# An attention kernel with two MLP layers: the flag of an all-masked row moves from GpSimd to VectorE

## The chip, the cores and the metric

The program runs on one core of a Trainium2 chip. The core has four engines that compute: TensorE multiplies and transposes matrices, VectorE and ScalarE read the results and work on rows, and GpSimd works on the core's memory beside them. SyncE issues transfers. The metric is the device time of one execution in microseconds (us).

## The reference

What is computed, in order: attention over 4 × 8 heads, 576 positions and 64 columns, in which each row keeps only the scores within `tau` of its maximum, and then two MLP layers over 2304 tokens.

```python
def _attn_ref(q, k, v, tau):
    scale = 1.0 / np.sqrt(q.shape[-1])
    scores = scale * np.matmul(q, k.transpose(0, 1, 3, 2))
    thresh = np.max(scores, axis=-1, keepdims=True) - tau
    scores = np.where(scores >= thresh, scores, -1000000000.0)
    scores = scores - np.max(scores, axis=-1, keepdims=True)
    attn = np.exp(scores)
    attn = attn / (np.sum(attn, axis=-1, keepdims=True) + 1e-09)
    return np.matmul(attn, v).astype(np.float32)

def _moe_ref(x, w_in, w_out, s, b):     # 512 -> 2048 -> 512
    h = x @ w_in
    r = np.maximum(h, 0.0)
    return (s * (r * r) + b) @ w_out

def _moe2_ref(x, w_in, w_out, alpha):   # 512 -> 2048 -> 512
    h = x @ w_in
    g = np.maximum(h, 0.0) + alpha * np.minimum(h, 0.0)
    return g @ w_out
```

A row in which nothing passes the threshold would be a row of equal weights in the reference, since all its scores are then the same. The kernel covers that case with a flag: where the sum of a row is zero, a small number is added to each of its entries before the division.

## The kernel before

The program has three stages: attention, then the first and the second MLP layer. Each engine has a program of its own in one block, and semaphores tie them together. There is no scheduler: the order on each engine is the order in which its code is written.

**Attention** goes over 16 pairs of heads. A pair has 9 tiles of 128 query rows by 576 keys: tile 0 to 7 belong to one head each, even ones to the first and odd ones to the second, and tile 8 holds the last 64 rows of both. `LAYOUT = ["Q", 0, 1, "K", 2, 3, "L", 4, 5, 6, 7, 8]` gives the 12 positions of a pair: at "Q" and "K" the next pair's q and k are transposed, at "L" the last tile of the pair before. `steps` calls each engine's `emit` once per position; pairs 0, 1, 14 and 15 are written out, pairs 2 to 13 run in a loop of two pairs. In the loop the counts that waits compare with are computed in registers of the engine.

A tile passes through five steps. TensorE puts its scores into one of three double banks (`fill`). VectorE takes the negated row maximum (`row_max`, line 788). ScalarE computes the exponentials into `ex` (`exp`, line 616), GpSimd the threshold (`threshold`, line 537). VectorE masks the exponentials with the threshold and sums each row into `rsum` (`mask`, line 796); its semaphore `freed` gives the double bank back to TensorE. For every two tiles (and for tile 8 alone), VectorE adds the guard to the sums (`denominator`, line 802, `den`), inverts them (`invert`, line 807, `rinv`), and GpSimd computes the flag (`all_masked`, line 544, `none_in`). GpSimd then normalises each tile in place (`normalise`, line 550), three positions behind the scores. TensorE transposes the normalised tiles (line 1038, tails in 1035, the last tile in 1046), ScalarE copies them out (line 638), and TensorE multiplies them with v (lines 1072 and 1067). VectorE and ScalarE also split q and k into a high and a low part (`qk_low`, line 814, and line 627).

`all_masked` waits for two things: that the normalisation nine tiles earlier is done, because it overwrites a column of `none_in` that this one read, and that the masking which closes the pair of tiles is done. `normalise` waits for the flag (`none_ok`) and for the inverse (`rinv_ok`). `wait` attaches a wait to the instruction that follows; `wait_alone` puts it on an instruction of its own, which also counts up the semaphore `tick`.

At one position GpSimd normalises, then computes the next threshold, then the flag. VectorE takes the next row maximum, the denominator, a low part of q or k where there is one, masks, and inverts.

The MLP layers follow from some 293 us on. They don't use `none_in`.

Of the kernel before, what the change touches and what calls it, by code (L numbers as in the profile page):

```python
# [28 lines left out]
ALU = mybir.AluOpType  # L29
# [3 lines left out]
P = 128  # L33
# [4 lines left out]
def attention_mlp_mlp(nc, q, k, v, tau, w_in1, w_out1, s, b, w_in2, w_out2, alpha, out):  # L38
    B, H, S, D = q.shape
# [10 lines left out]
    FULL = 2 * (QT - 1)  # L50
    TPP = FULL + 1
# [15 lines left out]
    with ExitStack() as whole, ExitStack() as attention_memory:  # L67
        def sb(name, shape, dt=F32, where=whole):
            return where.enter_context(nc.sbuf_tensor(name, shape, dt))

        def sem(name):
            return whole.enter_context(nc.semaphore(name))
# [39 lines left out]
        none_in = sb("none_in", [P, TPP], where=att)  # L112
        rsum = sb("rsum", [P, TPP], where=att)
# [42 lines left out]
        freed = sem("freed")  # L156
# [5 lines left out]
        none_ok = sem("none_ok")  # L162
        den_ok = sem("den_ok")
        rinv_ok = sem("rinv_ok")
        normed = sem("normed")
# [23 lines left out]
        def wait(eng, sm, value):  # L189

            if not (isinstance(value, int) and value <= 0):
                eng.wait_ge(sm, value)

        def wait_alone(eng, sm, value):

            if not (isinstance(value, int) and value <= 0):
                eng.wait_ge(sm, value)
                eng.sem_inc(tick, 1)
# [10 lines left out]
        GUARD = 1e-9  # L209
# [41 lines left out]
        WEIGHTS += [("in2", j) for j in range(FC)]  # L251
        WEIGHTS += [("out2", j) for j in range(FC)]
        STAGED = [m for m, (kind, _) in enumerate(WEIGHTS) if kind != "in1"]

        def split(kind, j):
# [93 lines left out]
        def last_tile(i):  # L349

            return Use(FINAL - 1, POS + LAYOUT.index(i))
# [10 lines left out]
        def steps(eng, emit):  # L362


            for l in range(-5, BODY):
                emit(0, l)
            with eng.Fori(1, PAIRS // 2 - 1) as it:
                for l in range(BODY):
                    emit(it * 2, l)
            for l in range(BODY):  # L370
                emit(PAIRS - 2, l)
# [136 lines left out]
        @block.gpsimd  # L508
        def _(pool):
            nc.gpsimd.memset(ident[:], 0.0).then_inc(ident_ok, 1)  # L510
            pool.wait_ge(ident_ok, 1)
            nc.gpsimd.affine_select(out=ident[:], in_=ident[:], compare_op=ALU.not_equal, fill=1.0, base=0,
                                    pattern=[[-1, P]], channel_multiplier=1).then_inc(ident_ok, 1)
            nc.gpsimd.memset(q_diag_lo[:].bitcast(F32), 0.0).then_inc(diag_padded, 1)
            pool.wait_ge(tau_in, DMA)
            nc.gpsimd.tensor_scalar(ntau_c[:], tau_c[:], -1.0, 0.0, ALU.mult, ALU.add).then_inc(consts_ok, 1)
            pool.wait_ge(consts_ok, 1)

            def split_lo(m):
                kind, j = WEIGHTS[m]  # L520
                pool.wait_ge(w_hi_ok, m + 1)
                if kind[:2] == "in":
                    chunk = win_lo[:, :, j * P:(j + 1) * P]
                    src = win_raw[:, :, j * P:(j + 1) * P]
                    if kind == "in2":
                        src = stage[:, STAGED.index(m) % 4, :].rearrange("p (c f) -> p c f", c=DC)
                    nc.gpsimd.tensor_tensor(chunk, src, win_hi[:, :, j * P:(j + 1) * P].bitcast(F32),
                                            ALU.subtract).then_inc(w_ok, 1)
                else:
                    nc.gpsimd.tensor_tensor(wout_lo[:, j, :], stage[:, STAGED.index(m) % 4, :],  # L530
                                            wout_hi[:, j, :].bitcast(F32), ALU.subtract).then_inc(w_ok, 1)

            def threshold(t):

                r, c = slice(0, P), t.col
                wait_alone(pool, maxed, t.count + 1)
                nc.gpsimd.tensor_scalar(thr[r, c], negm[r, c], -1.0, ntau_c[r, :], ALU.mult, ALU.add).then_inc(thr_ok, 1)

            def all_masked(t):

                r, c = slice(0, P), t.cols
                wait_alone(pool, normed, t.count - TPP + 1)
                wait_alone(pool, freed, t.uses + 1)
                nc.gpsimd.tensor_scalar(none_in[r, c], rsum[r, c], 0.0, GUARD / S, ALU.is_le, ALU.mult).then_inc(none_ok, 1)

            def normalise(t):
                r, c = slice(0, P), t.col
                wait_alone(pool, none_ok, t.twos + 1)
                wait_alone(pool, rinv_ok, t.twos + 1)
                nc.gpsimd.tensor_scalar(t.ex, t.ex, none_in[r, c], rinv[r, c], ALU.add,  # L550
                                        ALU.mult).then_inc(normed, 1)

            def emit(n0, l):
                before, after, normed_now = Use(n0, l - 1), Use(n0, l + 1), Use(n0, l - NORM_LAG)
                if normed_now.tile:
                    normalise(normed_now)
                if after.tile:
                    threshold(after)
                if before.tile and before.closes:
                    all_masked(before)  # L560

            steps(pool, emit)
            all_masked(last_tile(FULL))
            normalise(last_tile(FULL - 2))
            for m in range(IN1_AHEAD):
                split_lo(m)
            pool.wait_ge(o_out, 2 * PAIRS)
            for m in range(IN1_AHEAD, len(WEIGHTS)):
                split_lo(m)
# [214 lines left out]
        def _(dve):  # L784
# [14 lines left out]
            def denominator(t):  # L799
                r, c = slice(0, P), t.cols  # L800
                wait(dve, freed, t.uses + 1)
                nc.vector.tensor_scalar(den[r, c], rsum[r, c], GUARD, None, ALU.add).then_inc(den_ok, 1)

            def invert(t):
                r, c = slice(0, P), t.cols
                wait(dve, den_ok, t.twos + 1)
                nc.vector.reciprocal(rinv[r, c], den[r, c]).then_inc(rinv_ok, 1)  # L807
# [19 lines left out]
            def emit(n0, l):  # L827
                before, t, after = Use(n0, l - 1), Use(n0, l), Use(n0, l + 1)
                if after.tile:
                    row_max(after)  # L830
                if before.tile and before.closes:
                    denominator(before)
                if t.prepares:
                    qk_low(t)
                if t.tile:
                    mask(t)
                if before.tile and before.closes:
                    invert(before)

            steps(dve, emit)  # L840
            denominator(last_tile(FULL))
            invert(last_tile(FULL))
            for t in (last_tile(FULL - 1), last_tile(FULL)):
                dve.wait_ge(none_ok, t.twos + 1)
# [360 lines left out]
```

## Time and profile before

| | us |
|---|---|
| median of 3 runs | 1107.29 |
| lowest and highest | 1106.79, 1107.41 |
| the profiled execution | 1107.03 |
| its span, first to last instruction | 1105.1 |
| TensorE busy in the span | 1090.8 (99%) |
| VectorE busy | 525.6 (48%) |
| ScalarE busy | 507.9 (46%) |
| GpSimd busy | 258.0 (23%) |

The granted TensorE clock is 0.998 of full over the span. A busy share is a mean over stages that differ: in attention four engines are in use at once, in the MLP layers TensorE is nearly alone. Starts are counted from the first instruction of the span. The row of an instruction ends with the idle time of its engine before it and what ended that, where there was one. Matrix products overlap, so gaps of TensorE show in the rows of its weight loads (PEld) rather than in those of its products (PE). VectorE's rows overlap by some 0.08 us too: a row's duration reaches beyond the start of the next one.

### The profile page before, as it was taken

How to read it: one execution, taken by the hardware profiler on the slowest of the kernel's cores; microseconds unless marked ns; L12 is line 12 of the kernel's file. 1: busy time of each engine (PE TensorE's matmuls, PEld its weight loads, DVE VectorE, ACT ScalarE, POOL GpSimd, SP SyncE). 2: the span in 40 equal slices, each digit the busy share in tenths (PEclk: the TensorE clock that was granted, in tenths of full speed). 3: DMA queues.
4: the chain of work that ended last, by engine and by line, in shares of the span. 5: the costliest groups of instructions: out<-in, count | busy, mean ns of one | idle time of the engine just before them, and what ended most of it. 6: DMA issues, size and time to landing. Idle time of an engine off the chain costs nothing.

```text
span 1105.1 us, 18966 instructions
## 1 busy us (share of the span) xinstructions
PE 1090.8 (99%) x5826; PEld 892.2 (81%) x5826; DVE 525.6 (48%) x1016; ACT 507.9 (46%) x946; POOL 258.0 (23%) x438
## 2 busy tenths in 40 slices
PE   8999999999999999999999999999999999999998
PEld 7777877777688888888888889888888888888897
DVE  7888889888643332242242246522322332332232
ACT  4777878777654332232232235544433333333343
POOL 3566656566564300000000004322000000000000
PEclk9999999999999999999999999999999999999999
DMA  8666566664121100000000003311100100010010
GB/s 188 153 157 154 141 150 149 153 146 123 31 58 48 48 1 1 1 0 0 0 0 0 0 10 96 86 48 29 39 0 0 38 0 0 0 38 0 0 39 20
DMA packets 86554, 59.28 MB, mean 54 GB/s; under 512 B 49376, under 2 KB 69872, under 8 KB 86512
## 3 DMA queue, kind: packets, MB, share of 16 engines
q1 hardware_dynamic: 83248, 57.58, 20.5%
q10 hardware_dynamic: 3264, 1.18, 0.5%
q8 instruction: 22, 0.36, 0.1%
q14 instruction: 20, 0.16, 0.1%
HBM read 30.94 MB, written 4.72 MB: 32 GB/s over the span
## 4 chain that ended last, share of the span: by engine, by line
PE 93%; DVE 2%; ACT 2%; issue 1%; DMA 0%; POOL 0%; SPq 0%; ACTq 0%; POOLq 0%; DVEq 0%
PE psum L938 23%; PE psum L940 23%; PE psum L939 23%; PE psum L1072 6%; PE psum L1038 5%; PE psum L967 3%; PE psum L969 3%; PE psum L951 2%; PE psum L1067 2%; DVE act_r L874 2%; PE psum L1046 1%; ACT win_hi L593 1%; PE psum L1035 1%; ACT act_r L706 0%; DMA k_twice<-k_hi 0%
## 5 line engine op out<-in xcount | busy, mean ns | idle before, releaser
L940 PE MATMUL psum<-x_hi,win_lo 128*128 128x512 f32 (+1 forms) x640 | 238.7, 373 | 0.0
L939 PE MATMUL psum<-x_lo,win_hi 128*128 128x512 f32 (+1 forms) x640 | 238.2, 372 | 0.0
L938 PE MATMUL psum<-x_hi,win_hi 128*128 128x512 f32 (+1 forms) x640 | 238.1, 372 | 0.0
L939 PEld LDWEIGHTS psum<-x_lo,win_hi 128*128 128x128 f32 x640 | 120.2, 188 | 24.0
L938 PEld LDWEIGHTS psum<-x_hi,win_hi 128*128 128x128 f32 x640 | 120.3, 188 | 23.0
L940 PEld LDWEIGHTS psum<-x_hi,win_lo 128*128 128x128 f32 x640 | 120.2, 188 | 22.9
L885 DVE SCALAR_TENSOR_TENSOR act_r<-act_n,nalpha,act_r 128x512 f32<-128x512 f32 (+1 forms) x80 | 56.2, 702 | 160.1 <-ACT act_r L717 159.8
L874 DVE SCALAR_TENSOR_TENSOR act_r<-act_r,s_c 128x512 f32<-128x512 f32 (+1 forms) x80 | 72.4, 905 | 116.4 <-ACT act_r L706 116.4
L616 ACT ACTIVATE ex<-psum,negm 128x576 f32<-128x576 f32 x144 | 107.5, 747 | 37.9 <-DVE negm L788 36.7
L709 ACT ACTIVATE g_hi<-act_r,b_c 128x512 fp32r<-128x512 f32 (+1 forms) x80 | 54.6, 682 | 152.5 <-PE psum L940 122.4
L550 POOL TENSOR_SCALAR ex<-ex,none_in,rinv 128x576 f32<-128x576 f32 x142 | 117.5, 828 | 19.9 <-DVE rinv L807 13.0
L796 DVE SCALAR_TENSOR_TENSOR ex<-psum,thr,ex 128x576 f32<-128x576 f32 x144 | 117.1, 813 | 8.8 <-ACT ex L616 3.7
L788 DVE TENSOR_REDUCE negm<-psum 128x1 f32<-128x576 f32 x144 | 107.8, 748 | 25.7 <-PE psum L969 24.1
L877 DVE SCALAR_TENSOR_TENSOR g_lo<-act_r,b_c,g_hi 128x512 fp32r<-128x512 f32 (+1 forms) x80 | 56.4, 704 | 133.6 <-ACT g_hi L709 133.6
L938 PE MATMUL psum<-g_hi,wout_hi 128*128 128x512 f32 (+1 forms) x320 | 118.1, 369 | 1.0 <-DVE g_lo L877 1.0
L940 PE MATMUL psum<-g_hi,wout_lo 128*128 128x512 f32 (+1 forms) x320 | 118.1, 369 | 0.0
L939 PE MATMUL psum<-g_lo,wout_hi 128*128 128x512 f32 (+1 forms) x320 | 117.7, 368 | 0.0
L940 PE MATMUL psum<-wout_hi,g_lo 128*128 128x512 f32 x288 | 112.6, 391 | 0.0
L938 PE MATMUL psum<-wout_hi,g_hi 128*128 128x512 f32 x288 | 112.4, 390 | 0.0
L939 PE MATMUL psum<-wout_lo,g_hi 128*128 128x512 f32 x288 | 112.2, 390 | 0.0
L888 DVE TENSOR_TENSOR g_lo<-act_r,g_hi 128x512 fp32r<-128x512 f32 (+1 forms) x80 | 51.1, 639 | 105.8 <-ACT g_hi L720 105.8
L716 ACT ACTIVATE act_n<-psum 128x512 f32<-128x512 f32 (+1 forms) x80 | 44.3, 554 | 120.7 <-PE psum L940 120.7
(93 smaller groups left out, 1614.7 us busy)
## 6 DMA issues: line engine op xcount, KB each, us to landing
k_twice<-k_hi SPq DMA_DIRECT2D x64, 144.0 KB, 2.5
stage<-in_moe_w_out_dram SPq DMA_DIRECT2D x32, 256.0 KB, 2.6
out_dram<-stage SPq DMA_DIRECT2D x18, 256.0 KB, 2.2
q_both<-q_hi SPq DMA_DIRECT2D x32, 128.0 KB, 2.3
q_both<-q_lo SPq DMA_DIRECT2D x32, 128.0 KB, 2.3
win_raw<-in_moe_w_in_dram SPq DMA_DIRECT2D x16, 256.0 KB, 2.9
stage<-in_moe_w_in_dram SPq DMA_DIRECT2D x16, 256.0 KB, 2.6
raw_q<-in_q_dram SPq DMA_DIRECT2D x30, 128.0 KB, 2.4
```

What stands on the lines that cost most here:

```text
L550: nc.gpsimd.tensor_scalar(t.ex, t.ex, none_in[r, c], rinv[r, c], ALU.add, ALU.mult).then_inc(normed, 1)
L616: nc.scalar.activation(t.ex.rearrange("p (a c) -> p a c", a=2), t.wide[r, :, 0:HALF], ACT.Exp, bias=negm[r, t.col]).then_inc(exped, 1)
L788: nc.vector.tensor_reduce(negm[r, t.col], t.wide[r, :, 0:HALF], AX.XY, ALU.max, negate=True).then_inc(maxed, 1)
L796: nc.vector.scalar_tensor_tensor(out=e, in0=t.wide[r, :, 0:HALF], scalar=thr[r, t.col], in1=e, op0=ALU.is_ge, op1=ALU.mult, accum_out=rsum ...
L874: nc.vector.scalar_tensor_tensor(out=r, in0=r, scalar=s_c[:], in1=r, op0=ALU.mult, op1=ALU.mult).then_inc(t_ok, 1)
L877: nc.vector.scalar_tensor_tensor(out=g_lo[:, j % 2, 0:n], in0=r, scalar=b_c[:], in1=g_hi[:, j % 2, 0:n].bitcast(F32), op0=ALU.add, op1=ALU ...
L885: nc.vector.scalar_tensor_tensor(out=r, in0=act_n[:, j % 2, 0:n], scalar=nalpha[:, j:j + 1], in1=r, op0=ALU.mult, op1=ALU.add).then_inc(t_ ...
L938: nc.tensor.matmul(dst, lhs[0], rhs[0], start=first, stop=False)
L939: nc.tensor.matmul(dst, lhs[0], rhs[1], start=False, stop=False)
L940: return nc.tensor.matmul(dst, lhs[1], rhs[0], start=False, stop=final)
L1038: mm = nc.tensor.transpose(t.buf[:, c, :], ex[:, t.keys0 + c * P:t.keys0 + (c + 1) * P], ident[:])
L1072: nc.tensor.matmul(o_bank[part, o_cols], raw_v[:, par, h, c, :], pt[:, h, c, cols], start=(c == 0), stop=False)
```

## The change

The flag is computed by VectorE, right behind the denominator, instead of by GpSimd at the end of its position. The operation, its inputs and its shape stay: 128 × 2 elements, or 128 × 1 for tile 8. Both waits move with it.

```diff
@@ -536,13 +536,6 @@
-            def all_masked(t):
-
-                r, c = slice(0, P), t.cols
-                wait_alone(pool, normed, t.count - TPP + 1)
-                wait_alone(pool, freed, t.uses + 1)
-                nc.gpsimd.tensor_scalar(none_in[r, c], rsum[r, c], 0.0, GUARD / S, ALU.is_le, ALU.mult).then_inc(none_ok, 1)
-
...
                     threshold(after)
-                if before.tile and before.closes:
-                    all_masked(before)
 
             steps(pool, emit)
-            all_masked(last_tile(FULL))
             normalise(last_tile(FULL - 2))
@@ -801,6 +791,13 @@
+            def all_masked(t):
+
+                r, c = slice(0, P), t.cols
+                wait_alone(dve, normed, t.count - TPP + 1)
+                wait(dve, freed, t.uses + 1)
+                nc.vector.tensor_scalar(none_in[r, c], rsum[r, c], 0.0, GUARD / S, ALU.is_le, ALU.mult).then_inc(none_ok, 1)
+
...
                 if before.tile and before.closes:
                     denominator(before)
+                    all_masked(before)
                 if t.prepares:
                     qk_low(t)
...
             denominator(last_tile(FULL))
+            all_masked(last_tile(FULL))
             invert(last_tile(FULL))
```

VectorE, at the end of a pair inside the loop, before the change: the masking of tile 7, the denominator of tiles 6 and 7, the masking of tile 8, the inverse, then the next pair's row maximum of tile 0, the denominator of tile 8 and the low part of q. REGISTER_ALU and ISA are instructions of the engine's queue alone.

```order
L796 SCALAR_TENSOR_TENSOR ex,rsum<-psum,thr,ex 128x576 [waits thr_ok,exped]
L802 TENSOR_SCALAR den<-rsum 128x2 [waits freed]
L197 REGISTER_ALU
L796 SCALAR_TENSOR_TENSOR ex,rsum<-psum,thr,ex 128x576 [waits thr_ok,exped]
L192 REGISTER_ALU
L807 RECIPROCAL rinv<-den 128x2 [waits den_ok]
L192 ISA
L788 TENSOR_REDUCE negm<-psum 128x1 [waits filled]
L802 TENSOR_SCALAR den<-rsum 128x1 [waits freed]
L192 ISA
L814 SCALAR_TENSOR_TENSOR q_lo<-psum,q_hi 128x576 [waits qk_hi_ok]
```

The same place with the change (its line numbers are those of the changed file):

```order
L786 SCALAR_TENSOR_TENSOR ex,rsum<-psum,thr,ex 128x576 [waits thr_ok,exped]
L792 TENSOR_SCALAR den<-rsum 128x2 [waits freed]
L197 REGISTER_ALU
L799 TENSOR_SCALAR none_in<-rsum 128x2 [waits normed,freed]
L197 REGISTER_ALU
L786 SCALAR_TENSOR_TENSOR ex,rsum<-psum,thr,ex 128x576 [waits thr_ok,exped]
L192 REGISTER_ALU
L804 RECIPROCAL rinv<-den 128x2 [waits den_ok]
L192 ISA
L778 TENSOR_REDUCE negm<-psum 128x1 [waits filled]
L792 TENSOR_SCALAR den<-rsum 128x1 [waits freed]
L799 TENSOR_SCALAR none_in<-rsum 128x1 [waits normed,freed]
```

Between the denominator and the masking of tile 8 there are now the flag with its two waits and one more register instruction, and the flag of tile 8 stands before the low part of q.

GpSimd at the same place before the change: the normalisation of tile 5, the flag of tiles 6 and 7, the normalisation of tile 6, the next pair's threshold of tile 0, the flag of tile 8, the normalisation of tile 7.

```order
L550 TENSOR_SCALAR ex<-ex,none_in,rinv 128x576 [waits none_ok,rinv_ok]
L197 REGISTER_ALU
L197 REGISTER_ALU [waits normed]
L544 TENSOR_SCALAR none_in<-rsum 128x2 [waits freed]
L197 REGISTER_ALU
L550 TENSOR_SCALAR ex<-ex,none_in,rinv 128x576 [waits none_ok,rinv_ok]
L197 ISA
L537 TENSOR_SCALAR thr<-negm,ntau_c 128x1 [waits maxed]
L197 REGISTER_ALU [waits normed]
L544 TENSOR_SCALAR none_in<-rsum 128x1 [waits freed]
L550 TENSOR_SCALAR ex<-ex,none_in,rinv 128x576 [waits none_ok,rinv_ok]
```

With the change:

```order
L543 TENSOR_SCALAR ex<-ex,none_in,rinv 128x576 [waits none_ok,rinv_ok]
L197 REGISTER_ALU
L543 TENSOR_SCALAR ex<-ex,none_in,rinv 128x576 [waits none_ok,rinv_ok]
L197 ISA
L537 TENSOR_SCALAR thr<-negm,ntau_c 128x1 [waits maxed]
L543 TENSOR_SCALAR ex<-ex,none_in,rinv 128x576 [waits none_ok,rinv_ok]
```

The three normalisations have only the threshold between them now.

## Rows read from the trace of the kernel before

**Rows 1.** Windows: length, busy of PE, PEld, DVE, ACT, POOL, clock, DMA share, GB/s.

```profile
140.00:180.00 40.00, 39.69 (x288) 30.85 (x286) 35.19 (x88) 30.41 (x58) 24.26 (x52) 1.00 0.62 149
...
400.00:1105.00 705.00, 700.08 (x3317) 582.74 (x3315) 233.21 (x336) 239.47 (x448) 41.54 (x32) 1.00 0.06 17
```

**Rows 2.** Timeline, ScalarE copy of the last turned tile: start, duration, engine, line.

```profile
36.23 0.59 ACT L643 COPY pt<-psum 128x512 f32<-128x512 f32 x1 [1.09 <-PE psum L1046]
...
265.30 0.59 ACT L643 COPY pt<-psum 128x512 f32<-128x512 f32 x1 [1.05 <-PE psum L1046]
```

**Rows 3.** Waits of weight loads, 60 to 260 us: total, times, longest.

```profile
PEld psum L1038 <- issue: 4.1, 12, 0.4
```

**Rows 4.** Timeline of one period's end, 147.3 to 155.7 us, all engines.

```profile
147.39 0.76 DVE L788 TENSOR_REDUCE negm<-psum 128x1 f32<-128x576 f32 x1 [0.92 <-PE psum L969]
...
148.13 0.81 DVE L796 SCALAR_TENSOR_TENSOR ex<-psum,thr,ex 128x576 f32<-128x576 f32 x1
...
148.94 0.74 DVE L788 TENSOR_REDUCE negm<-psum 128x1 f32<-128x576 f32 x1
149.00 0.53 PEld L951 LDWEIGHTS psum<-ident,raw_q 128*128 128x128 f32 x5 [0.22 <-DVE ex L796]
...
149.24 0.82 POOL L550 TENSOR_SCALAR ex<-ex,none_in,rinv 128x576 f32<-128x576 f32 x1 [0.32 <-DVE rinv L807]
...
149.59 0.81 DVE L796 SCALAR_TENSOR_TENSOR ex<-psum,thr,ex 128x576 f32<-128x576 f32 x1
...
149.71 0.74 ACT L616 ACTIVATE ex<-psum,negm 128x576 f32<-128x576 f32 x1
150.15 0.26 POOL L537 TENSOR_SCALAR thr<-negm,ntau_c 128x1 f32<-128x1 f32 x1
...
150.40 0.83 POOL L550 TENSOR_SCALAR ex<-ex,none_in,rinv 128x576 f32<-128x576 f32 x1
150.45 0.17 DVE L802 TENSOR_SCALAR den<-rsum 128x2 f32<-128x2 f32 x1
...
150.66 0.82 DVE L796 SCALAR_TENSOR_TENSOR ex<-psum,thr,ex 128x576 f32<-128x576 f32 x1
...
151.48 0.74 DVE L788 TENSOR_REDUCE negm<-psum 128x1 f32<-128x576 f32 x1
...
152.19 0.75 DVE L814 SCALAR_TENSOR_TENSOR q_lo<-psum,q_hi 128x576 fp32r<-128x576 f32 x1
...
152.77 0.27 POOL L537 TENSOR_SCALAR thr<-negm,ntau_c 128x1 f32<-128x1 f32 x1
...
152.92 0.74 DVE L788 TENSOR_REDUCE negm<-psum 128x1 f32<-128x576 f32 x1
...
153.12 0.23 POOL L544 TENSOR_SCALAR none_in<-rsum 128x1 f32<-128x1 f32 x1
...
153.33 0.82 POOL L550 TENSOR_SCALAR ex<-ex,none_in,rinv 128x576 f32<-128x576 f32 x1
...
153.75 0.77 ACT L616 ACTIVATE ex<-psum,negm 128x576 f32<-128x576 f32 x1
154.25 0.27 POOL L537 TENSOR_SCALAR thr<-negm,ntau_c 128x1 f32<-128x1 f32 x1
...
154.42 0.42 PEld L1038 LDWEIGHTS psum<-ident,ex 128*128 128x128 f32 x4 [0.35 <-issue]
...
154.66 0.82 DVE L796 SCALAR_TENSOR_TENSOR ex<-psum,thr,ex 128x576 f32<-128x576 f32 x1 [0.26 <-POOL thr L537]
...
155.56 0.19 PEld L967 LDWEIGHTS psum<-k_twice,q_both 128*128 128x128 f32 x1
```

**Rows 5.** The flag's tile `none_in`: count, duration in ns least, median and greatest.

```profile
L544 POOL TENSOR_SCALAR none_in<-rsum x80: 218/219/238, 16.1 to 292.5; 128x2 f32<-128x2 f32 x64, 128x1 f32<-128x1 f32 x16
```

**Rows 6.** Timeline, tiles 6 and 7 of pair 1, written out without the loop.

```profile
44.67 0.17 DVE L802 TENSOR_SCALAR den<-rsum 128x2 f32<-128x2 f32 x1
...
44.80 0.82 DVE L796 SCALAR_TENSOR_TENSOR ex<-psum,thr,ex 128x576 f32<-128x576 f32 x1
```

## The prediction

> **What bounds the kernel now.** I read the windows by stage first, then the starts that give the attention period, the waits of the weight loads, and one period instruction by instruction. The windows split the span in two [rows 1]. After 400 us, in the two MLP layers, TensorE is busy for 700 of 705 us and nothing that the edit touches runs any more. The edit acts only in attention, up to some 293 us. There VectorE is busy 35.2 of 40 us, ScalarE 30.4, GpSimd 24.3, and TensorE is shown as busy for 39.7, although its weight loads, which show the gaps better, fill 30.9.
>
> Attention repeats once per pair of heads: the copies of the last turned tile start at 36.23 and 265.30 us, with twelve between them, so 13 periods last 229.07 us, 17.62 us each [rows 2]. The waits of the weight loads name a wait of 4.1 us in 12 times, 0.34 each, before transposes of line 1038, put down to "issue" [rows 3]. I take it for a wait on GpSimd: the normalisation of tile 7 runs from 153.33 to 154.15, and the load starts 0.27 us later, at 154.42 [rows 4]. Before the q transposes at 149.00 TensorE waits 0.22 us for a masking on VectorE.
>
> So four engines lean on each other, and a cost on any counts only as far as it reaches TensorE. VectorE is the one with least room: between the row maximum of tile 7 at 147.39, which waited 0.92 us for TensorE, and the masking of tile 1 of the next pair at 154.66 no row of it carries an idle time [rows 4].
>
> **What is taken away.** 80 GpSimd instructions of 219 ns [rows 5], 17.5 us of an engine with room. On the path it matters in one place: the flag of tile 8 at 153.12 stands between the threshold at 152.77 and the normalisation of tile 7 at 153.33. Without it the latter follows the threshold by 0.25 us, as at 150.15 and 150.40, so at 153.02: 0.31 us earlier. The normalisations of tiles 4 and 6 wait for rinv (the row at 149.24 says so) and gain nothing from it; those of tile 2 may, but no wait of TensorE hangs on them. What would TensorE do with 0.31 us? It would start tile 7's transposes earlier, then the scores of tiles 2 and 3. But the bank for tile 3 comes free only when tile 1 is masked, 154.66 + 0.82 = 155.48; with the 0.06 us from such an end to the load (tile 6's masking ends at 148.94, the q load starts at 149.00) that allows 155.54, and the load of tile 3 starts at 155.56. **The gain is 0.02 us per pair**, because the masking of tile 1 waits for the exponential as much as for GpSimd: that ends at 153.75 + 0.77 = 154.52, and the threshold at 154.25 + 0.27 = 154.52 too.
>
> **What is added.** 80 VectorE instructions of the shape of den, and before each a separate wait on `normed` with its count. That wait asks for the normalisation nine tiles back, while GpSimd runs three uses behind: it will find it done. What counts is the time that the next VectorE instruction loses. In a period there are five places.
> - Flags of tiles 4 and 5. The row max takes 0.74 us from its start to the next start where den lies between (147.39 to 148.13), 0.65 where it doesn't (148.94 to 149.59); 0.02 of it is the longer row max. A small instruction queued behind a long one costs **0.07 us**.
> - Flag of tile 8, before q_lo: 151.48 to 152.19 is 0.71, so **0.06 us**.
> - Flags of tiles 6 and 7. Here den is not queued: it waits for the masking of tile 7 (149.59 to 150.40), starts at 150.45, and the masking of tile 8 starts only at 150.66, **0.21 us** later. The data were there sooner: the exponential of tile 8 ends at 150.45, the threshold at 150.41, and at tile 1 the masking followed both 0.14 us after their end. In the part written out without a loop the same pair of starts is 0.13 apart [rows 6]; in the loop the order has a register instruction between. I read the 0.21 as the time in which VectorE's queue works through register, wait and masking once den has let it go, with no long instruction to cover it. The flag brings one more register instruction, one more wait and itself, the same form. Bounds: 0 if only data held the masking back, 0.21 if the row repeats. I take **0.21**, the row nearest in form; 0.13 where no register is computed.
> - Tiles 2 and 3: between den and rinv, which has to wait for den anyway; nothing. Tiles 0 and 1: 0.07, swallowed by VectorE's next wait for TensorE.
>
> **The path, in the loop.** The row max of tile 7 stays at 147.39, it starts with TensorE. Everything after it moves by 0.07, from tile 8's masking on by 0.28 (150.94), and from q_lo on by 0.34. So the row max of tile 1 ends at 153.66 + 0.34 = 154.00, and its exponential, which ScalarE started at 153.75 behind its own queue, starts 0.03 us after that (as 149.71 behind 149.68): 154.03, 0.28 later. The masking of tile 1 follows, 154.94, frees the bank at 155.76, and tile 3's load starts at 155.82 in place of 155.56: **+0.26 us per pair**. The k transposes start later by up to 0.34 too, since q_lo (152.19 + 0.75 = 152.94) holds their bank. But behind them lie the 0.35 us of waiting for tile 7, and these take it up: the normalisation of tile 7 moves by 0.28 with rinv and by 0.31 the other way. From tile 3 on TensorE's stream is gapless or waits for work that it started itself, so that the 0.26 stays until the next period.
>
> **Sum.** The loop holds the ends of pairs 2 to 13: 12 × 0.26 = 3.1. The written-out ends of pairs 1 and 14: 0.07 + 0.13 + 0.06 − 0.08 = 0.18 each, 0.4 (the 0.08 is what ScalarE's queue and the bank leave: 0.34 against 0.26). The end of pair 0 is free, VectorE waits for TensorE there. At the end of attention the exponential of the last tile moves by 0.07. With rounding **+3.5 us**: span 1105.1 to 1108.6, its own run 1107.03 to 1110.6; the run shown lies 0.3 under the median 1107.29, hence **1110.8**.
>
> **Rivals.**
> - *The flag hides in the queue* (nothing at tiles 6 and 7). For it: in all other places register and wait instructions are not seen. Against: 0.21 in the loop, 0.13 outside. Then 0.07 + 0.06 = 0.13 reaches the row max of tile 1, 0.07 its exponential, 0.05 TensorE; 14 × 0.05 + 0.07 = 0.8: 1108.1.
> - *The relief of GpSimd pays.* If ScalarE could start tile 1's exponential some 0.2 us sooner, TensorE would win up to the 0.2 us by which tile 7 comes sooner once VectorE's own 0.13 is paid: 14 × 0.2 = 2.8, 1104.5. It decides from the point where that exponential ends before 154.3. Against it: ScalarE's rows from 149.71 to 154.52 touch each other.
> - *Each flag costs its full slot*, 0.21 in all three places, queued or not: 0.63 − 0.08 = 0.55 a pair, 14 × 0.55 = 7.7: 1115.
> - *The flag and the normalisation exclude each other.* If VectorE had to wait for a normalisation under way, tiles 6 and 7 would lose until 151.23, and tile 8 about 0.5: some 1.07 a pair, 15 us, 1122. Against it: den, the same operation and shape, starts at 150.45 inside the normalisation of 150.40 and takes 0.17, the normalisation 0.83 in place of 0.82. No row shows that den runs in the mode that the flag would run in, so a little chance stays. The Trainium skill has this as a rule (SBUF — State Buffer, "Who interferes with whom"): a VectorE tensor_scalar can take both ports, and then it or the GpSimd instruction, whichever comes second, blocks fully. By that rule the time would be this rival's; the row of den speaks against it here.
>
> **Chances.** Forecast 0.51, hidden 0.27, relief pays 0.07, full slot 0.12, exclusion 0.03. What a measurement of this kernel can tell from no change is about 0.2%, 2.2 us: under 1105.1 is faster, over 1109.5 slower. The forecast case has its own range of 1109.3 to 1111.5, with 0.04 under the line. Slower 0.47 + 0.12 + 0.03 = 0.62; same 0.27 + 0.04 = 0.31; faster 0.07. The range takes in the hidden case with its spread and the lower half of the full slot, 1107.3 to 1113.5, and leaves 0.07 below and about 0.1 above.
>
> **What will show it.** Period 17.88 in place of 17.62; den of tiles 6 and 7 to masking of tile 8 0.4 in the loop, den to masking of tile 6 0.14; the wait before tile 7's transposes near zero; a wait of a load of line 967 for a masking at tile 3, some 0.3 us; GpSimd 17.5 us less busy; the part after 300 us unchanged in length. If the 0.4 reads 0.21, the hidden case holds; if ScalarE's exponential of tile 1 moves by less than VectorE's row max, the price is smaller than summed. A longer normalisation beside a flag would speak for exclusion.

## The result, and the profile after

The changed kernel takes 1111.56 us in the median of 5 runs (1111.47 to 1112.21), against 1107.29 before: a ratio of 1.0042, 95% interval 1.0031 to 1.0052, so it is slower by some 4.3 us. Its profiled execution has a span of 1109.8 us, 4.7 more than that of before. Of the runs below one of e5's five took 1788.52 us, at a granted clock of 0.556; without it the median of e5 would be 1111.7 in place of 1111.91.

The part behind attention did not change. The conversion of x that opens it starts at 299.20 us and the span ends 810.6 us later; before the same two were 294.54 and again 810.6 apart. So all of the difference lies in the attention pairs. The windows of after (columns as in [rows 1]) show the move in the first stretch: VectorE 0.9 us busier in 40, GpSimd 2.8 less, while TensorE and ScalarE lose share because the period got longer.

```profile
140.00:180.00 40.00, 39.32 (x286) 30.56 (x286) 36.07 (x98) 29.87 (x57) 21.47 (x40) 1.00 0.63 151
400.00:1105.00 705.00, 704.00 (x3335) 586.30 (x3334) 234.95 (x339) 241.01 (x450) 41.57 (x32) 1.00 0.05 17
```

The period is read from the starts of q_lo on VectorE, one per pair: 17.63 us before (12 periods of 17.60 to 17.71), 17.99 after (all 13 between 17.97 and 18.02). That is **+0.36 us a pair** where the prediction had +0.26. The same twelve periods make 4.3 of the 4.7 us; at their start q_lo already comes 0.4 us later than before, from the first pairs.

The tiles of the small instructions come next: line, engine, operation and count, then least, median and greatest duration in ns. The flag itself is a 160 ns instruction on VectorE, never longer than 165. But `den`, which the change doesn't touch, has a greatest duration of 706 ns, where it was 172 before.

```profile
L799 DVE TENSOR_SCALAR none_in<-rsum x80: 134/160/165, 14.8 to 297.6; 128x2 f32<-128x2 f32 x64, 128x1 f32<-128x1 f32 x16
L792 DVE TENSOR_SCALAR den<-rsum x80: 133/158/706, 14.7 to 297.5; 128x2 f32<-128x2 f32 x64, 128x1 f32<-128x1 f32 x16
```

Here is the timeline of the period's end that answers to [rows 4]; row 149.37 is the row maximum of tile 7, at 147.39 before.

```profile
149.37 0.76 DVE L778 TENSOR_REDUCE negm<-psum 128x1 f32<-128x576 f32 x1 [1.07 <-PE psum L968]
...
150.04 0.16 DVE L792 TENSOR_SCALAR den<-rsum 128x2 f32<-128x2 f32 x1
150.11 0.16 DVE L799 TENSOR_SCALAR none_in<-rsum 128x2 f32<-128x2 f32 x1
150.18 0.81 DVE L786 SCALAR_TENSOR_TENSOR ex<-psum,thr,ex 128x576 f32<-128x576 f32 x1
...
152.09 0.27 POOL L537 TENSOR_SCALAR thr<-negm,ntau_c 128x1 f32<-128x1 f32 x1
...
152.34 0.83 POOL L543 TENSOR_SCALAR ex<-ex,none_in,rinv 128x576 f32<-128x576 f32 x1
...
152.49 0.69 DVE L792 TENSOR_SCALAR den<-rsum 128x2 f32<-128x2 f32 x1
...
153.09 0.16 DVE L799 TENSOR_SCALAR none_in<-rsum 128x2 f32<-128x2 f32 x1
...
153.16 0.81 DVE L786 SCALAR_TENSOR_TENSOR ex<-psum,thr,ex 128x576 f32<-128x576 f32 x1
...
154.26 0.84 POOL L543 TENSOR_SCALAR ex<-ex,none_in,rinv 128x576 f32<-128x576 f32 x1 [1.10 <-DVE rinv L804]
...
154.63 0.14 DVE L792 TENSOR_SCALAR den<-rsum 128x1 f32<-128x1 f32 x1
154.69 0.14 DVE L799 TENSOR_SCALAR none_in<-rsum 128x1 f32<-128x1 f32 x1
154.75 0.74 DVE L811 SCALAR_TENSOR_TENSOR q_lo<-psum,q_hi 128x576 fp32r<-128x576 f32 x1
...
155.48 0.73 DVE L778 TENSOR_REDUCE negm<-psum 128x1 f32<-128x576 f32 x1
155.54 0.64 PEld L950 LDWEIGHTS psum<-ident,raw_k 128*128 128x128 f32 x6 [0.51 <-DVE q_lo L811]
...
156.25 0.74 ACT L606 ACTIVATE ex<-psum,negm 128x576 f32<-128x576 f32 x1 [0.29 <-DVE negm L778]
...
157.02 0.82 DVE L786 SCALAR_TENSOR_TENSOR ex<-psum,thr,ex 128x576 f32<-128x576 f32 x1
...
157.90 0.19 PEld L966 LDWEIGHTS psum<-k_twice,q_both 128*128 128x128 f32 x1
```

Three readings. The den of tiles 6 and 7 (row 152.49) starts 0.15 us after the normalisation of tile 5 (152.34) and lasts 0.69 us: it ends at 153.18, and the normalisation at 153.17. Before, it started 0.05 us after it, and took 0.17 [rows 4]. One-column den and flag of tile 8 (154.63, 154.69) lie deeper still, 0.37 and 0.43 us, in the normalisation of 154.26 and take 0.14. And the wait of the weight loads before tile 7's transposes, 0.34 us a pair in [rows 3], has gone; the loads now wait for q_lo before the k transposes (row 155.54).

How far each step came from tile 7's row maximum, before and after: masking of tile 8 3.27 and 3.79 (+0.52); q_lo 4.80 and 5.38 (+0.58); row maximum of tile 1 5.53 and 6.11 (+0.58); its exponential 6.36 and 6.88 (+0.52); its masking 7.27 and 7.65 (+0.38); tile 3's load 8.17 and 8.53 (+0.36).

The traces hold one more place where the two engines meet, at the very end of attention, where VectorE normalises two tiles of 128 × 576 itself while GpSimd normalises a third. First the kernel before, then the changed one:

```profile
292.60 1.07 DVE L846 TENSOR_SCALAR ex<-ex,none_in,rinv 128x576 f32<-128x576 f32 x2
292.74 1.46 POOL L550 TENSOR_SCALAR ex<-ex,none_in,rinv 128x576 f32<-128x576 f32 x1
```

```profile
297.77 1.13 POOL L543 TENSOR_SCALAR ex<-ex,none_in,rinv 128x576 f32<-128x576 f32 x1 [1.10 <-DVE rinv L804]
297.79 1.42 DVE L845 TENSOR_SCALAR ex<-ex,none_in,rinv 128x576 f32<-128x576 f32 x2
```

A VectorE row stands for both of its instructions. Before, VectorE starts 0.14 us ahead: its two take 0.58 each, and GpSimd's takes 1.46 in place of 0.82. After, GpSimd's recorded start is 0.02 ahead: VectorE's first takes 0.58 all the same and GpSimd's 1.13; VectorE's second, 0.52 behind GpSimd's start, takes 0.93. So the two engines already held each other up in the kernel before, once, and either can be the one that is held.

### The profile page after: what moved, and what is told of

The parts are those of the page before. It is cut to its first block, busy times and chain, and to the rows that moved or that the text cites. A ratio compares the mean times of both kernels' runs of the same rounds, so it can differ in the third digit from the quotient of the medians.

```text
span 1109.8 us, 18826 instructions
## 1 busy us (share of the span) xinstructions
PE 1093.1 (99%) x5826; PEld 893.5 (81%) x5826; DVE 535.9 (48%) x1096; ACT 508.7 (46%) x946; POOL 240.1 (22%) x358
## 4 chain that ended last, share of the span: by engine, by line
PE 85%; DVE 6%; issue 4%; ACT 1%; SPq 1%; DVEq 1%; DMA 0%; POOL 0%; ACTq 0%; POOLq 0%
PE psum L939 23%; PE psum L937 23%; PE psum L938 23%; PE psum L1071 6%; PE psum L966 3%; PE psum L968 2%; PE psum L1066 2%; DVE act_r L873 2%; PE psum L1037 2%; DVE ex L786 1%; PE psum L950 1%; DVE negm L778 1%; PE psum L1045 1%; DVE q_lo L811 1%; ACT win_hi L583 1%
```

## The experiments

Two theories stood after this. **Hold** (exclusion in the expectations)**:** a two-column tensor_scalar of VectorE that starts well inside a normalisation on GpSimd is held until that ends; the 0.52 us is this. **Queue:** the flag's register and wait instructions on VectorE cost what the prediction said, and den's length only covers them. The table has all kernels; the period is the mean from the q_lo starts, the ratio is to the kernel before on the same chip.

| kernel | median us (runs) | ratio (95%) | period us |
|---|---|---|---|
| after | 1111.56 (5) | 1.0042 (1.0031 to 1.0052) | 17.99 |
| e1_den_single | 1111.40 (5) | 1.0040 (1.0026 to 1.0055) | 17.96 |
| e2_both_single | 1111.95 (4) | 1.0043 (1.0026 to 1.0060) | 17.98 |
| e3_no_flags | 1108.55 (10) | 1.0015 (1.0005 to 1.0024) | 17.79 |
| e4_spare_on_vector | 1114.27 (4) | 1.0066 (1.0049 to 1.0083) | 18.13 |
| e5_no_normed_wait | 1111.91 (5) | 1.0044 (1.0028 to 1.0060) | 17.98 |
| e6_behind_mask | 1112.25 (4) | 1.0047 (1.0030 to 1.0064) | 18.01 |
| e7_single_no_wait | 1107.65 (10) | 1.0006 (0.9996 to 1.0016) | 17.69 |
| e8_before_behind_mask | 1112.66 (4) | 1.0053 (1.0036 to 1.0070) | 18.04 |
| e9_no_flags_single_67 | 1105.02 (11) | 0.9985 (0.9976 to 0.9994) | 17.49 |
| e10_single_67 | 1106.22 (11) | 0.9993 (0.9984 to 1.0002) | 17.57 |
| e11_before_single_67_nowait | 1106.82 (11) | 1.0000 (0.9991 to 1.0009) | 17.62 |

### What holds den

**e1**, after with den issued one column at a time:

```diff
-                nc.vector.tensor_scalar(den[r, c], rsum[r, c], GUARD, None, ALU.add).then_inc(den_ok, 1)
+                for i in range(c.start, c.stop):
+                    one = nc.vector.tensor_scalar(den[r, i:i + 1], rsum[r, i:i + 1], GUARD, None, ALU.add)
+                one.then_inc(den_ok, 1)
```

> The changed kernel, but each denominator of two tiles is issued as two instructions of one column; the flag stays two columns wide. Exclusion theory (a two-column tensor_scalar on VectorE that starts 0.15 us into a GpSimd normalisation waits for its end): den no longer has the row of 0.69 us at tiles 6 and 7, but the flag right behind it, two columns wide, takes its place with a row of 0.5 to 0.6 us, so the period stays near 17.98 and the time near 1111.5. Queue-work theory (register, wait and flag cost 0.21 us between den and masking): no row over 0.2 us, one small instruction more, period some 18.0 to 18.1.

Its timeline at the same place:

```profile
152.17 0.83 POOL L543 TENSOR_SCALAR ex<-ex,none_in,rinv 128x576 f32<-128x576 f32 x1
...
152.33 0.21 DVE L793 TENSOR_SCALAR den<-rsum 128x1 f32<-128x1 f32 x2
152.54 0.48 DVE L801 TENSOR_SCALAR none_in<-rsum 128x2 f32<-128x2 f32 x1
152.93 0.81 DVE L786 SCALAR_TENSOR_TENSOR ex<-psum,thr,ex 128x576 f32<-128x576 f32 x1
```

The two one-column den start 0.16 us into the normalisation and are not held (x2, 0.21 together). The flag, still two columns wide, is held in their place and ends with the normalisation, at 153.02 and 153.00. So it is the shape that decides, not den as such. The time is that of the changed kernel, as that theory expected.

**e3**, the kernel before with the flag's computation left out: `none_in` is set to zero once, so a row that is masked throughout gets no uniform weights. GpSimd has its whole relief and VectorE nothing added.

```diff
+            nc.gpsimd.memset(none_in[:], 0.0).then_inc(none_ok, 1)
...
-                wait_alone(pool, none_ok, t.twos + 1)
...
-                if before.tile and before.closes:
-                    all_masked(before)
```

> The kernel before without any computation of the flag: none_in is set to zero once at the start, the waits for none_ok are gone, VectorE's order is that of before. It measures GpSimd's relief alone. By the prediction's working the relief is worth 0.02 us a pair: period 17.60, 1107.0. Exclusion theory: the relief brings the normalisation of tile 5 some 0.1 us nearer to the den of tiles 6 and 7 from the front, to 0.15 us ahead of it, and den then waits about 0.5 us with no flag on VectorE at all: period 17.9, 1110 to 1111. Queue-work theory: period 17.6, no long row.

```profile
150.79 0.83 POOL L551 TENSOR_SCALAR ex<-ex,none_in,rinv 128x576 f32<-128x576 f32 x1
...
150.95 0.69 DVE L800 TENSOR_SCALAR den<-rsum 128x2 f32<-128x2 f32 x1
151.55 0.80 DVE L794 SCALAR_TENSOR_TENSOR ex<-psum,thr,ex 128x576 f32<-128x576 f32 x1
```

This is the plainest run of the study. Less work was done than in the kernel before, and it took 1.6 us longer. From tile 7's row maximum (147.89) den starts 3.06 us on, as before; the normalisation 2.90 us on, where it was 3.01. GpSimd came 0.11 us sooner, the distance went from 0.05 to 0.16, and den was held for half a microsecond. No flag on VectorE is needed for that. The hold came as expected; its price didn't, 17.79 in place of 17.9, because the relief of GpSimd pays elsewhere (e9, below).

**e4**, the kernel before with the flag's instruction and its two waits added on VectorE, where it writes a tile `spare` that nobody reads; the real flag stays on GpSimd.

```diff
+            def spare_flag(t):
+                r, c = slice(0, P), t.cols
+                wait_alone(dve, normed, t.count - TPP + 1)
+                wait(dve, freed, t.uses + 1)
+                nc.vector.tensor_scalar(spare[r, c], rsum[r, c], 0.0, GUARD / S, ALU.is_le, ALU.mult)
...
                     denominator(before)
+                    spare_flag(before)
```

> The kernel before, flags still on GpSimd, plus the flag's instruction with both its waits on VectorE at the place of the change, writing to a tile of its own that nobody reads. It measures VectorE's load alone. Queue-work theory: the row pair den to masking of tile 8 goes from 0.21 to 0.42, period 17.88, 1110.8. Exclusion theory: den and the normalisation of tile 5 shift together, den stays 0.05 us behind its start and is not held, so the period moves only by the small instructions, 17.65 to 17.8, 1107.8 to 1109.5; if the spare flag itself, 0.1 us later, is held, it shows a row of 0.5 us instead and the period is near 17.98.

```profile
153.38 0.83 POOL L551 TENSOR_SCALAR ex<-ex,none_in,rinv 128x576 f32<-128x576 f32 x1
153.43 0.17 DVE L803 TENSOR_SCALAR den<-rsum 128x2 f32<-128x2 f32 x1
153.64 0.60 DVE L809 TENSOR_SCALAR spare<-rsum 128x2 f32<-128x2 f32 x1
154.15 0.80 DVE L797 SCALAR_TENSOR_TENSOR ex<-psum,thr,ex 128x576 f32<-128x576 f32 x1
```

Both cases stand in one normalisation. den, 0.05 us behind its start, takes 0.17; the same shape 0.26 us behind it takes 0.60, to 154.24, when the normalisation has ended (154.21). Between them lie the 0.21 us that the prediction had read as the queue's work on register and wait. The spare flag is held as one of the expectations had it, but the period is 18.13 and not 17.98: here GpSimd keeps its flags, and 0.14 is what their absence is worth in e9.

### Whether the queue's work costs too

**e2** is e1 with the flag one column at a time as well. **e5** is after without `wait_alone(dve, normed, t.count - TPP + 1)`, the order between flag and normalisation nine tiles back being left to the other waits. **e7** is e2 and e5 together. Nothing is left out of the result in any of them.

> The changed kernel with denominator and flag both issued one column at a time (45 instructions turn into 80 for each in kind, all narrow). Exclusion theory: a single column never waits for a normalisation (rows of tile 8 take 0.14 us in the midst of one), so no row over 0.2 us is left; what remains is the cost of small instructions, 0.07 us each on VectorE, period 17.65 to 17.8, time 1107.5 to 1109.5. Queue-work theory: two more uncovered instructions between den and masking, period 18.1 or more, 1113.

> The changed kernel without the separate wait on normed (the masking's wait on the threshold, which GpSimd computes behind those normalisations, still orders the two). It takes one wait and one register instruction from VectorE's queue per flag. If the hold of den alone sets the distance, den still shows its row of 0.69 us at tiles 6 and 7 and the period stays at 17.98, 1111.5. If queue work sets it, den to masking of tile 8 falls from 0.67 to 0.5 or less, period 17.85, 1109.5.

> Denominator and flag one column at a time and no separate wait on normed: neither a hold nor the extra queue work. The kernel of single columns had 0.58 us from den to the masking of tile 8, with 0.32 of it between the last den and the first flag where the register and wait instructions stand. Both theories together: that gap shrinks to about 0.06 to 0.1, den to masking to 0.35 to 0.45, period 17.75 to 17.85, 1108.5 to 1109.5. If only the hold mattered, it would be as the kernel of single columns: 17.96, 1111.5.

The same place in e2, then e5, then e7:

```profile
152.94 0.82 POOL L543 TENSOR_SCALAR ex<-ex,none_in,rinv 128x576 f32<-128x576 f32 x1
...
153.10 0.21 DVE L793 TENSOR_SCALAR den<-rsum 128x1 f32<-128x1 f32 x2
153.42 0.22 DVE L802 TENSOR_SCALAR none_in<-rsum 128x1 f32<-128x1 f32 x2
153.68 0.82 DVE L786 SCALAR_TENSOR_TENSOR ex<-psum,thr,ex 128x576 f32<-128x576 f32 x1
```

```profile
152.02 0.82 POOL L543 TENSOR_SCALAR ex<-ex,none_in,rinv 128x576 f32<-128x576 f32 x1
...
152.18 0.69 DVE L792 TENSOR_SCALAR den<-rsum 128x2 f32<-128x2 f32 x1
152.78 0.15 DVE L798 TENSOR_SCALAR none_in<-rsum 128x2 f32<-128x2 f32 x1
152.85 0.80 DVE L786 SCALAR_TENSOR_TENSOR ex<-psum,thr,ex 128x576 f32<-128x576 f32 x1
```

```profile
150.86 0.21 DVE L793 TENSOR_SCALAR den<-rsum 128x1 f32<-128x1 f32 x2
150.99 0.21 DVE L801 TENSOR_SCALAR none_in<-rsum 128x1 f32<-128x1 f32 x2
151.11 0.81 DVE L786 SCALAR_TENSOR_TENSOR ex<-psum,thr,ex 128x576 f32<-128x576 f32 x1
```

Read the distance from den to the masking of tile 8, with the period behind it:

| | with the wait | without the wait |
|---|---|---|
| two columns (held) | after: 0.67, 17.99 | e5: 0.67, 17.98 |
| one column (not held) | e2: 0.55, 17.98 | e7: 0.25, 17.69 |

The 0.55 of e2 is the mean of the loop's twelve pairs: 0.47 and 0.58 by turns, once 0.83. Taking away the wait alone gains nothing; taking away both gains 0.30 us a pair and 4 us in all. The two lie in the same time: while den is held, VectorE's queue works through what belongs to the flag's wait; where den isn't held, that work stands bare. In the pair of e2 shown it is 0.32 us from den to flag, 0.13 in e7, and 0.26 from flag to masking, 0.12 in e7. Most of it comes with the count that the loop computes in a register, not with the wait itself: in pairs 1, 14 and 15, which are written out, e2 has the wait with a fixed count, and goes from den to flag in 0.13 and to the masking in 0.31. Pair 1, where the masking starts at 45.68:

```profile
45.37 0.21 DVE L793 TENSOR_SCALAR den<-rsum 128x1 f32<-128x1 f32 x2
45.50 0.21 DVE L802 TENSOR_SCALAR none_in<-rsum 128x1 f32<-128x1 f32 x2
```

That e2 comes out level with the changed kernel is in part chance: 0.12 us a pair are won here, and some 0.1 is lost before, where the extra small instructions at tiles 4 and 5 put den 3.23 us behind tile 7's row maximum in place of 3.12. No kernel takes the hold out of the changed one at tiles 6 and 7 alone and leaves the wait. What the hold costs with no flag's wait in play is read from e3 and e9: 17.79 against 17.49.

Neither theory's range held e2 (17.65 to 17.8, or 18.1 and more). e5 came as the hold had it, 17.98, with the row of 0.69. e7 came 0.06 us under its range.

### Another place for the pair

**e6** puts den and flag behind the masking instead of before it; **e8** does that to den in the kernel before.

```diff
-                if before.tile and before.closes:
-                    denominator(before)
-                    all_masked(before)
                 if t.prepares:
                     qk_low(t)
                 if t.tile:
                     mask(t)
                 if before.tile and before.closes:
+                    denominator(before)
+                    all_masked(before)
                     invert(before)
```

> The changed kernel with denominator and flag issued behind the masking instead of in front of it, right before the inverse. The masking of tile 8 then follows that of tile 7 without small instructions, and den starts some 0.8 us later, when the normalisation of tile 5 ends. Exclusion theory: no row of den or flag over 0.2 us at tiles 6 and 7. The price is that the inverse now waits openly for den, about 0.1 to 0.15 us at each of the places on the path. Sum: 0.5 us won at the masking of tile 8, 0.3 to 0.4 lost up to the row max of tile 1: period 17.75 to 17.9, 1108 to 1110.5. Queue-work theory: the same sign, 0.2 us won, period 18.0 to 18.1.

> The kernel before (flags on GpSimd) with the denominator behind the masking, right before the inverse. Den was not held in the kernel before (0.17 us), so the exclusion theory gives no gain from the hold; the masking of tile 8 comes up to 0.1 us sooner, the inverse waits openly for den, some 0.1 us at each place, and the flags on GpSimd are unaffected. Period 17.6 to 17.8, 1107 to 1109.5. It tells how much of the result of the same order in the changed kernel is the order and how much the flag.

Neither den is held, and both kernels are the slower for it. The inverse then waits openly for den (156.71 to 156.91 in e6, where it used to lie a whole masking behind), and at the loop's end the row maximum waits as well. The row of e6, then that of e8:

```profile
157.42 0.76 DVE L778 TENSOR_REDUCE negm<-psum 128x1 f32<-128x576 f32 x1 [0.34 <-issue]
```

```profile
154.28 0.76 DVE L788 TENSOR_REDUCE negm<-psum 128x1 f32<-128x576 f32 x1 [0.34 <-issue]
```

Since e8 has no flag on VectorE and reads the same 0.34, the loss is the order's. Such a row comes at every second pair, where the loop of two pairs goes round, and the periods go up and down with it: 17.83 and 18.23 to 18.28 in e6, 17.85 to 17.89 and 18.25 to 18.30 in e8. So what the masking otherwise covers there is queue work of the loop's end; which instructions of it take the time isn't settled. Both expectations were missed, by 0.1 and 0.2 us a pair: they had priced the open wait of the inverse and not this. The profiled execution of e6 is its longest, 1115.18, and its first pairs, which the period leaves out, are up to 2 us longer than the rest.

### What each part is worth, and a better version

**e9** is e3 with den of tiles 6 and 7 in single columns (the flag's computation again left out). **e10** is after with den and flag of these two tiles in single columns and without the normed wait: the whole computation. **e11** is the kernel before with the same two edits, its flag still on GpSimd, as is the wait. The edit of e10, but for the flag's columns, which are split like den's:

```diff
-                wait_alone(dve, normed, t.count - TPP + 1)
...
+                den_of = [slice(i, i + 1) for i in range(c.start, c.stop)] if t.i == 7 else [c]
+                for cols in den_of:
+                    one = nc.vector.tensor_scalar(den[r, cols], rsum[r, cols], GUARD, None, ALU.add)
+                one.then_inc(den_ok, 1)
```

> As the kernel without any flags (none_in zero from the start), with the denominator of tiles 6 and 7 issued one column at a time and nothing else changed. There den of two columns was held for 0.69 us and the period was 17.79. If the hold was the whole loss of that kernel, no den row over 0.22 us is left, the relief of GpSimd shows its own worth, and the period is 17.55 to 17.62, 1106 to 1107 (the prediction had 0.02 us a pair for it). If something else in the lighter GpSimd queue cost the 0.17 us a pair, the period stays near 17.79, 1108.5.

> The changed kernel without the separate wait on normed, denominator and flag one column at a time at tiles 6 and 7 only, two columns wide elsewhere. The kernel that had this everywhere ran a period of 17.69. No hold is possible at the one place where a normalisation is under way, and two small instructions of 0.06 us less lie on the path at tiles 4 and 5: period 17.60 to 17.68, 1106.8 to 1107.6, level with the kernel before. If a hold turns up at another place, the period is 17.9 or more.

> The kernel before, flags on GpSimd, without GpSimd's own separate wait on normed in front of the flag, and the denominator of tiles 6 and 7 one column at a time, so that a normalisation that starts sooner can't hold it. GpSimd's queue gets lighter without anything moving to VectorE. Path reasoning: at most 0.02 us a pair is to be won before the bank of tile 3, against 0.06 for the extra small instruction, which the masking's wait for the exponential may cover: period 17.58 to 17.66, 1106.5 to 1107.7. A lighter GpSimd queue that cost by itself would show as 17.75 or more.

The end of the period in e9, tile 1's exponential, threshold and masking:

```profile
152.49 0.77 ACT L614 ACTIVATE ex<-psum,negm 128x576 f32<-128x576 f32 x1
152.62 0.27 POOL L539 TENSOR_SCALAR thr<-negm,ntau_c 128x1 f32<-128x1 f32 x1 [0.24 <-DVE negm L786]
...
153.29 0.82 DVE L794 SCALAR_TENSOR_TENSOR ex<-psum,thr,ex 128x576 f32<-128x576 f32 x1
...
154.17 0.19 PEld L968 LDWEIGHTS psum<-k_twice,q_both 128*128 128x128 f32 x1 [0.17 <-DVE ex L794]
```

With the hold out of the way the relief of GpSimd does pay, 0.14 us a pair (17.63 to 17.49). The exponential starts 6.36 us behind tile 7's row maximum (146.13), as before. But the masking follows its end, 153.26, by 0.03, where before it followed the threshold's end by 0.14 [rows 4]. A later threshold cost 0.11 us although both inputs ended at the same 154.52 in the record. The expectation had taken over the prediction's 0.02 for the relief and was missed: 17.49 and 1105.02 lie under its 17.55 and 1106.

Now the way from before to after can be cut into measured steps: relief −0.14 (before to e9), the flags as bare small instructions +0.08 (e9 to e10), hold and wait together +0.42 (e10 to after). That they make +0.36 follows from how they are cut; what is measured is the size of each. e10 is 5.3 us under after; against before, 0.9993, it can't be told apart, though its period is 0.06 shorter and both lie a little under what was expected. In e11, without relief, den stays 0.05 us behind the normalisation's start and the time is that of before, as expected. So the move of the flag, freed of what it ran into, brings 1106.22 against 1106.91, which isn't clear of noise; the interval leaves room for 1.8 us at most.

## Why the prediction was right, and where not

Direction and size came out: +3.5 us were forecast, +4.3 measured, inside the range. That is in part luck: the cause that it named for the greater part was not the one at work, and the time lies just above the forecast case's own 1109.3 to 1111.5.

- **The part behind attention, GpSimd's load, the wait before tile 7.** As said: 810.6 us in both, GpSimd 258.0 to 240.1 us busy (17.9 less, 17.5 forecast), the wait of [rows 3] gone.
- **Small instructions behind long ones.** 0.07 and 0.06 were forecast, 150.11 to 150.18 and 154.69 to 154.75 measured. Right.
- **Flags of tiles 6 and 7, the 0.21.** This step failed. The prediction let the den row stand at 0.17 and put another 0.21 behind it. What came is den itself, 0.52 longer in every pair but the first (0.36 there), and the flag behind it costs 0.07 (153.09 to 153.16). The queue's work is real (e2, e4: 0.21 to 0.32 from den to the next small instruction) but lies under the hold. That den to masking of tile 8 would read 0.4 was forecast; it reads 0.67. Outside the loop 0.13 was forecast to be added to den's 0.13; the rows below, pair 1, against [rows 6], show 0.68 in all.

```profile
44.51 0.70 DVE L792 TENSOR_SCALAR den<-rsum 128x2 f32<-128x2 f32 x1
45.12 0.16 DVE L799 TENSOR_SCALAR none_in<-rsum 128x2 f32<-128x2 f32 x1
45.19 0.81 DVE L786 SCALAR_TENSOR_TENSOR ex<-psum,thr,ex 128x576 f32<-128x576 f32 x1
```

- **The rival that two engines exclude each other**, given 0.03, is the mechanism that decided. It was argued away with one row, den at 150.45 inside the normalisation of 150.40. That row was 0.05 us behind a start. The same den is held at 0.15, and the argument never asked at what distance the row stood, nor that the edit would change the distance: den +0.06 from the flag of tiles 4 and 5 (3.06 to 3.12 from tile 7's row maximum), the normalisation 0.04 sooner from GpSimd's relief (3.01 to 2.97). That rival's own price, 1.07 a pair and 1122 us, was too high: of its two places only tiles 6 and 7 are held, tile 8's single columns are not, and of the 0.52 there only 0.36 arrives. The row that would have spoken for it stood in the trace of the kernel before: GpSimd's normalisation of 292.74, 1.46 us long beside VectorE's two. By the rule of the Trainium skill that the prediction cited (SBUF — State Buffer, "Who interferes with whom") the second comer blocks fully, and the trace agrees: every den or flag that is held ends within 0.03 us of the normalisation. The Trainium skill's condition for the mode that takes both ports (VectorE: DVE Perf Modes, "Mode 2×_2P") asks for an outermost non-unit dimension that is even, or odd and equal in source and destination; the two-column rows have an even one and are held, the one-column rows have none and aren't (e1). Of other widths the traces have only the 576 columns of attention's end, which are held too (0.93 in place of 0.58).
- **Relief worth 0.02.** Mis-sized: 0.14 in e9. The prediction had the masking of tile 1 bound by exponential and threshold alike, because both end at 154.52. The start behind a threshold is 0.14 later, behind an exponential 0.03.
- **The path from there.** It was forecast that VectorE's delay reaches tile 1's exponential with 0.06 taken off by ScalarE's queue: 0.58 to 0.52, exact. The next step gains 0.14 more, 0.11 of it by the trade just told and 0.03 by a shorter exponential (0.77 to 0.74). So two errors, a term 0.24 too small and a relief 0.12 too small, partly cancelled; +0.26 stood where +0.36 came. The last step holds: tile 3's load starts 0.06 behind the end of tile 1's masking (157.84 and 157.90). But the sign named for it, a wait of 0.3 us of line 967's load, doesn't show: from the start of the loads ahead of it 0.37 us pass (157.53 to 157.90), where it was 0.24 (155.32 to 155.56), and the waits of TensorE that grew are those for q_lo and for the masking ahead of the q transposes.
- **The hidden case** (1108.1) is excluded by e2 against e7: with nothing held, the wait and its register still cost 0.30 us a pair in the loop.
- **The full slot** (1115) is excluded by the rows: 0.07 and 0.06 at the two queued places, not 0.21. **The relief pays** came near in size (0.14 in e9, 0.2 in the rival), but not by its way: tile 1's exponential starts no sooner in e9, and VectorE's loss was the larger.

## What to carry to other kernels

Before work is moved between VectorE and GpSimd, look at every pair of their SBUF instructions that overlaps, and at the distance of their starts: a pair that goes well by 0.05 us may stop doing so from a shift of 0.1 us, even one that comes from less work (e3). A row that is used as proof that two things don't disturb each other is proof only for its own shape and its own distance. Where removing one suspected cause changes nothing (e5), remove both before either is cleared, and see that the edit which removes one adds nothing elsewhere (e2); and where two inputs end together, compare how late the start follows each of them.

## What the runs showed of the hardware

- A 128x2 float32 tensor_scalar on VectorE that starts 0.15 us or more behind the start of a 128x576 normalisation on GpSimd lasts until that one ends, in all 80 such rows of the traces within 0.03 us: 0.69 to 0.70 us at 0.15 to 0.17, 0.53 at 0.32 (pair 0 of after), 0.60 at 0.26 (e4), 0.48 at 0.37 (e1). At 0.02 to 0.06 it takes 0.17. The normalisation beside so small an instruction keeps its length (0.82 to 0.85). Distances between 0.06 and 0.15 did not occur for it.
- The hold goes both ways. A 128x576 normalisation on VectorE that starts 0.14 us ahead of one on GpSimd, followed by a second, makes GpSimd's 1.46 us in place of 0.82 (before). One whose recorded start is 0.02 us behind GpSimd's still isn't held (0.58), and GpSimd's takes 1.13 (after). So at so short a distance VectorE goes first; that this is also why den escapes at 0.05 fits, but isn't shown for den itself.
- A 128x1 tensor_scalar is never held, at 0.16 (e1), 0.36 or 0.42 us (after): none of the traces has one over 0.16 us beside a normalisation.
- A separate wait with a count computed in a register, before a small VectorE instruction, adds nothing behind a long one (0.07 us for flag and wait together, after). Where nothing covers it, it adds some 0.30 us from den to the masking: 0.55 in the loop of e2, 0.25 in e7. With a fixed count it adds 0.06: 0.31 in the written-out pairs of e2, 0.25 in those of e7.
- VectorE's masking starts 0.14 us behind the end of a GpSimd threshold that ended together with the exponential (before, both at 154.52), and 0.03 behind the end of a ScalarE exponential that came last (e9).
